# One wide instruction for two blocks: the high and low parts of blocks 1 and 2 of a group

## What is computed

```python
qn = q / (norm(q, axis=1) + 1e-06);  kn = k / (norm(k, axis=1) + 1e-06)
s = kn.transpose(0, 2, 1) @ qn / tau            # 256 x 256 for each b
a = softmax(s)                                  # row sums + 1e-9
x = (v @ a).reshape(B * N, C)
h = x @ w_in                                    # 12032 x 2048
g = maximum(h, 0) + alpha * minimum(h, 0)
y = g @ w_out                                   # 12032 x 256
```

## Time and profile before

| | |
|---|---|
| median of 3 runs | 1091.75 us (1090.86 to 1092.21) |
| the profiled execution | 1091.53 us |
| its span, first to last instruction | 1089.5 us |
| TensorE, matmuls busy | 1081.0 us (99%) |
| VectorE busy | 859.4 us (79%) |
| ScalarE busy | 648.1 us (59%) |
| granted clock of TensorE | 1.0 in all slices |

### The profile page before, as it was taken

One profiled execution on the slowest core, in us unless ns is written; L12 is line 12 of the kernel. 1 busy time (PEld: TensorE's weight loads), 2 busy tenths in 40 slices (PEclk: granted clock), 3 DMA queues, 4 the chain that ended last, 5 costly groups with the idle time before them and its releaser, 6 DMA issues.

```text
span 1089.5 us, 13668 instructions
## 1 busy us (share of the span) xinstructions
PE 1081.0 (99%) x4927; PEld 903.5 (83%) x4927; DVE 859.4 (79%) x1362; ACT 648.1 (59%) x1094; POOL 2.2 (0%) x9
## 2 busy tenths in 40 slices
PE   9999999999999999999999999999999999999998
PEld 7878788888887888788888888888888888888897
DVE  6889988778786787887888887887887887787675
ACT  6666667667666555655665655655655655655554
POOL 0000000000000000000000000000000000000000
PEclk9999999999999999999999999999999999999999
DMA  9620033443342101102101001101101101100100
GB/s 382 275 97 20 20 134 115 131 147 134 114 148 75 39 1 34 39 1 78 59 20 40 34 1 39 39 1 39 39 1 39 39 1 35 39 1 1 39 1 34
DMA packets 24499, 68.78 MB, mean 63 GB/s; under 512 B 2288, under 2 KB 7536, under 8 KB 22896
## 3 DMA queue, kind: packets, MB, share of 16 engines
q1 hardware_dynamic: 24432, 67.91, 17.5%
HBM read 55.58 MB, written 12.32 MB: 62 GB/s over the span
## 4 chain that ended last, share of the span: by engine, by line
PE 91%; DVE 4%; ACT 3%; issue 1%; DMA 1%; SPq 0%; ACTq 0%; DVEq 0%
PE y_ps L470 43%; PE x_ps L446 22%; PE z_ps L446 11%; PE p_ps L446 6%; PE x_ps L389 4%; PE s_ps L409 2%; PE p_ps L438 2%; DVE h L888 1%; ACT h L665 1%; DVE h L896 1%; DMA pair<-qk 1%; DVE g_lo L903 1%; ACT y_stage L687 0%; PE y_ps L485 0%; DMA stage<-qk 0%
## 5 line engine op out<-in xcount | busy, mean ns | idle before, releaser
L665 ACT ACTIVATE h<-x_ps,sigma 128x512 f32<-128x512 f32 (+1 forms) x384 | 261.3, 680 | 301.7 <-PE x_ps L446 288.7
L470 PE MATMUL y_ps<-g_hi,w_hi 128*128 128x512 f32 (+1 forms) x760 | 293.7, 386 | 0.0
L470 PE MATMUL y_ps<-g_hi,w_lo 128*128 128x512 f32 (+1 forms) x760 | 293.1, 386 | 0.0
L470 PE MATMUL y_ps<-g_lo,w_hi 128*128 128x512 f32 (+1 forms) x760 | 293.0, 386 | 0.0
L676 ACT CAST g_hi<-h 128x512 fp32r<-128x512 f32 (+1 forms) x384 | 234.0, 610 | 82.9 <-DVE h L896 75.7
L896 DVE SCALAR_TENSOR_TENSOR h<-h,small_sb 128x512 f32<-128x512 f32 (+1 forms) x384 | 273.9, 734 | 0.0
L888 DVE SCALAR_TENSOR_TENSOR h<-z_ps,sigma,h 128x512 f32<-128x512 f32 (+1 forms) x192 | 141.8, 738 | 148.6 <-ACT h L665 148.5
L903 DVE TENSOR_TENSOR g_lo<-h,g_hi 128x512 fp32r<-128x512 f32 (+1 forms) x384 | 250.2, 672 | 6.7 <-ACT g_hi L676 6.6
L470 PEld LDWEIGHTS y_ps<-g_hi,w_hi 128*128 128x128 f32 x760 | 142.6, 188 | 28.5 <-issue 1.1
L470 PEld LDWEIGHTS y_ps<-g_hi,w_lo 128*128 128x128 f32 x760 | 142.6, 188 | 27.2
L470 PEld LDWEIGHTS y_ps<-g_lo,w_hi 128*128 128x128 f32 x760 | 142.7, 188 | 26.9
(11 more groups left out here) (104 smaller groups left out, 891.1 us busy)
## 6 DMA issues: line engine op xcount, KB each, us to landing
rows_t<-qk_t SPq DMA_DIRECT2D x32, 376.0 KB, 3.5
stage<-qk SPq DMA_DIRECT2D x10, 1024.0 KB, 13.3
v_stage<-v_t SPq DMA_DIRECT2D x20, 512.0 KB, 4.6
y_t<-y_stage SPq DMA_DIRECT2D x20, 512.0 KB, 2.8
pair<-qk SPq DMA_DIRECT2D x19, 512.0 KB, 5.0
scratch<-w_in SPq DMA_DIRECT2D x12, 256.0 KB, 5.3
y_stage<-w_out SPq DMA_DIRECT2D x4, 512.0 KB, 7.4
v_stage<-v_t SPq DMA_DIRECT2D x4, 448.0 KB, 4.0
```

What stands on the lines that cost most here:

```text
L470: product = nc.tensor.matmul(y_ps[t][oc][:, 0:H], w_part[:, j, ws], g_part[:, k, 0:H], start=jp == 0 and k < 2 and w_part is w_hi and g_pa ...
L665: nc.scalar.mul(h[:, k, 0:H], X[:, 0:H], sigma[:, j:j + 1]).then_inc(x_copied, 1)
```

## The change

For all groups but the last one, the high parts of blocks 1 and 2 are made by one cast over both (2 x 512 columns, 2 x 448 in the narrow tiles), and their low parts by one subtraction. The cast waits until the slopes of blocks 0, 1 and 2 are done (`g_ready` 4 G + 3) and down(G-1, 2) too; the subtraction waits for both high parts. Each raises its semaphore by 2. What waits for these semaphores is as it was. The last group keeps its two and two.

```diff
+            def split_two_hi(G):
+
+                H = half_width(G // JP)
+                act.wait_ge(g_ready, 4 * G + 3)
+                if G > 0:
+                    act.wait_ge(down_done, 4 * (G - 1) + 3)
+                else:
+
+                    act.wait_ge(m_done, M_FIRST)
+                nc.scalar.copy(g_hi[:, 1:3, 0:H], h[:, 1:3, 0:H]).then_inc(g_hi_ready, 2)
...
-                for k in (1, 2) if G < GROUPS - 1 else (2, 1):
-                    split_g_hi(G, k)
+                if G < GROUPS - 1:
+                    split_two_hi(G)
+                else:
+                    for k in (2, 1):
+                        split_g_hi(G, k)
...
+            def split_two_lo(G):
+                H = half_width(G // JP)
+                dve.wait_ge(g_hi_ready, 4 * G + 3)
+                nc.vector.tensor_tensor(g_lo[:, 1:3, 0:H], h[:, 1:3, 0:H], g_hi[:, 1:3, 0:H].bitcast(fp32),
+                                        ALU.subtract).then_inc(g_lo_ready, 2)
...
-                for k in (1, 2) if G < GROUPS - 1 else (2, 1):
-                    split_g_lo(G, k)
+                if G < GROUPS - 1:
+                    split_two_lo(G)
+                else:
+                    for k in (2, 1):
+                        split_g_lo(G, k)
```

## The result

| | before | with the change |
|---|---|---|
| median | 1091.89 us (1090.86 to 1092.21, 4 runs) | 1098.28 us (1097.98 to 1099.31, 4 runs) |
| the profiled execution | 1091.53 us, span 1089.5 | 1099.31 us, span 1097.5 |

The ratio is 1.0062, with a 95% interval of 1.0044 to 1.0079: slower by 6.4 us where 1097.7 was forecast. The profiled execution is the slowest of the four and stands 1.0 above the median.

What follows compares the result with a forecast made beforehand. TensorE, busy 99% of the span, was taken as the bound. Delays in fourteen groups without a lead (3.34 + 0.83 + 0.43 + 1.48) sum to 6.08 us more, giving 1097.7 us, range 1094.5 to 1100.8.

Steps and rivals of the forecast that it cites:

- The bound: TensorE is busy 99% of the span, so time changes only where it waits or a longer wait elsewhere reaches it.
- The durations: Wide cast 1054 ns and wide subtraction 1219 ns, from existing rows of 1024 columns; 0.945 us for the 896-column cast.
- The bounds on both sides: Low: shorter wide forms, about 4.4 us more, 1095.9; high: as dear as two narrow ones, about 9.8 more, 1101.3.
- The delay on ScalarE: The wide cast starts when block 2's slope has ended, so ScalarE is free 0.43 us later in each group.
- The delay on VectorE: The subtraction starts 0.10 behind the wide cast's end, so VectorE is free 0.53 us later.
- The seams: Starts of tiles 4 to 11, without a lead: six at 0.43 us and two narrow at 0.38, 3.34 in all.
- Groups 34 and 35: Behind the pair ScalarE loads a table and the x load waits for its copy: 0.43 and 0.40, 0.83 us.
- The first tile: Groups 1 and 6 later by 0.53 us each, group 2 by 0.43, group 7 by 0.42; groups 3 to 5 covered.
- fewer instructions would bring time: Rival: one instruction fewer per group shortens the engines' round, 6.6 us on VectorE, 1085 us; 3%.
- half of it: Rival: only the seams or only the first tile lose time, 3 to 4 us, 1095; 10%.
- light groups open too: Rival: wide forms dearer by 0.5 us, some 70 light groups pay 0.1 each, 1104 or more; 7%.
- within 0.2%: Rival: the fourteen delays are cut to a third, 2 us, 1093.6; 7%.

Runs made afterwards that it cites:

- light_only: The change with wide pairs only where TensorE has a lead, 78 of 95 groups, narrow elsewhere, against the kernel before: 1092.0 us, ratio 0.9997.
- move_wide: The change with ScalarE's first two y copies at each seam ahead of the wide cast, against the kernel before: 1094.32 us, ratio 1.0022.
- wide_sub: Two narrow casts and the wide subtraction of the change, against the kernel before: 1092.53 us, ratio 1.0005.
- seams_only: Wide pairs only in the first group of tiles 4 to 11, narrow elsewhere, against the kernel before: 1095.21 us, ratio 1.0031.
- wide_cast: The wide cast of the change with two narrow subtractions, against the kernel before: 1099.13 us, ratio 1.0065.

## Why the prediction was right, point by point

**The bound.** TensorE's waits decide, and little else: as said. In the light groups the lateness is 0.27 at the add (0.22 was reckoned) and hidden. light_only shows it for 78 groups at once.

**The durations.** 1052 for 1054, 1225 for 1219, 944 for 945 in the narrow tiles. The bounds on both sides were not needed.

**The delay on ScalarE**, 0.43 reckoned, 0.47 measured. The two durations gave 0.43; the rest is that the cast now starts 0.82 behind the slopes' start and not 0.78. The narrow cast of block 2 also stood behind a shorter idle time (0.70, now 1.48), but the idle time is not the cause. At the seams of move_wide the wide cast stands behind 0.52 of it, and starts 0.82 behind the slopes all the same:

```profile
693.37 1.41 DVE L912 SCALAR_TENSOR_TENSOR h<-h,small_sb 128x512 f32<-128x512 f32 x2
...
694.19 1.05 ACT L687 CAST g_hi<-h 128x1024 fp32r<-128x1024 f32 x1 [0.52 <-issue]
```

So the 0.04 goes with the wide form; whether with its 1024 columns or its two blocks no run here tells.

**The delay on VectorE**, 0.53 reckoned, 0.60 measured, with the same 0.04 in it. It comes from the cast: wide_sub shows it.

**The seams**, 3.34 reckoned, 3.61 in the profile, 3.15 by the medians of seams_only. The reading of "issue" as `y_copied` was right: with the copies moved that wait is gone.

**Groups 34 and 35**, 0.83 reckoned, 0.88 measured. No run has these two alone; the profile of the change shows them, wide_cast has 0.47 and 0.38 there, and they are as before in the kernels where they are narrow.

**The first tile**, 1.91 reckoned, 2.55 measured. Here a step failed: "In the loaded groups 3 to 5 of the first tile VectorE is full; it has 0.67 idle left ... cost 0". The idle time ahead of the add of Z was counted as cover for VectorE's lateness, but what ends that idle time is ScalarE's copy of the x bank, and ScalarE is held up in turn by VectorE: its copy of m, just ahead, waits for `m_lo`, with a lead of 0.38 where 0.53 was to be covered. So the add comes 0.32 late with 0.29 of idle time left, and TensorE's second product into Z waits for it. TensorE's product for m waits for the add of Y besides, at about 0.1 in all. Together this cost 0.52 in the three groups, and 0.1 more in group 6, into which the rest was carried. Group 2 was shorter than reckoned (0.37 for 0.43).

**The sum.** 6.08 reckoned, 7.04 in the named groups of the profile, 6.4 by the medians. The forecast of 1097.7 is 0.6 below the median; most terms were a little low, by some 0.04 a place, and the first tile by the missed 0.6. That 6.08 lies 0.3 from the medians' 6.4 is partly luck: the sum misses that of the places by 0.96, and the interval of the measured ratio reaches from 4.8 to 8.6.

**The rivals.** That fewer instructions would bring time falls: 78 fewer on each engine bring nothing (light_only), and the rule of the Trainium skill ("Perfetto Trace Analysis", Optimizing Scalar/DVE Operations) says so itself with its condition "if the engine is saturated". VectorE is nearly that in the first tile (45.4 us busy of the 48 from 88 to 136 in the kernel before), and even there the wide subtraction alone made groups 1 and 6 longer, because it has to wait for both casts. The same section of the Trainium skill has the other rule, that breaking up instructions may allow work to be completed sooner where ScalarE or VectorE aren't saturated but cause bubbles on other engines. By the narrow and wide forms this case agrees: 1.05 us of work that could start only at the end of the wait, against 0.62. The rivals "half of it" and "light groups open too" are excluded by the profile, and "within 0.2%" by the interval, which begins at 0.44%.

## What to carry to other kernels

Two instructions made one start when the last input of both is there, and all of it is then still to do; the price is the part that used to be done by then, and the saved overhead (0.07 to 0.1 us here) is small beside it. Look for that price not in the average group but where the engine behind has no lead: the seams between tiles, a table load, a tile with extra work. To find all such places, go along the waiting engine's program wait by wait and take each releaser's end before its use. Then follow the releaser back: idle time of a late engine is cover only if what ends it does not itself wait for that engine. Here it did, by way of another engine, and time was lost with 0.29 us of the idle time still there.

## What was not expected of the hardware

Three small things. The wide cast starts 0.04 us later behind its releaser than the narrow one, after 1.48 us of idle time as after 0.52. The end of a load's wait for ScalarE's copy is called "issue" in one profile and laid to VectorE's `g_lo` in another, while the matmul's row names the copy. And of a nearly saturated engine the lateness doesn't all show at once: 0.10 us of it came out in a group whose own pair was narrow.
